# A fused attention and expert kernel: gate loads moved to ScalarE's queue, queries scaled ahead of the bonus sums, first keys decayed from PSUM, long idle products

## What is computed

```python
def _attn_ref(r, k, v, w, u):            # B, H, S, D = 4, 8, 768, 48
    state = zeros((B, H, D, D))
    for t in range(S):
        kt, vt, rt = k[:, :, t], v[:, :, t], r[:, :, t]
        cur = einsum('bhd,bhe->bhde', u[None] * kt, vt)
        y[:, :, t] = einsum('bhd,bhde->bhe', rt, state + cur)
        state = w[None, :, :, None] * state + einsum('bhd,bhe->bhde', kt, vt)

# x = y as 3072 tokens of 384. Expert layer: tokens with x @ w_skip > 0 go through
# the expert of their largest logit (x @ w_gate): x += gate * relu(x @ w1[e]) @ w2[e]
# Gated layer: out = ((x @ w1) * (x @ w2)) @ w3 @ w_out
```

## Time and profile before

| what | us |
|---|---|
| median of three runs | 617.81 |
| the profiled execution | 617.68 |
| its span, first to last instruction | 615.9 |
| TensorE busy (matmul rows) | 596.8 |
| VectorE, ScalarE, GpSimd busy | 292.5, 227.8, 144.7 |

### The profile page before, as it was taken

One profiled execution on the slowest core, in us unless ns is written; L12 is line 12 of the kernel. 1 busy time (PEld: TensorE's weight loads), 2 busy tenths in 40 slices (PEclk: granted clock), 3 DMA queues, 4 the chain that ended last, 5 costly groups with the idle time before them and its releaser, 6 DMA issues.

```text
span 615.9 us, 17326 instructions
## 1 busy us (share of the span) xinstructions
PE 596.8 (97%) x7377; PEld 532.8 (87%) x7377; DVE 292.5 (47%) x462; ACT 227.8 (37%) x409; POOL 144.7 (24%) x177
## 2 busy tenths in 40 slices
PE   6789999999999999999999999999999999999997
PEld 5689999766899999999688888888898888888886
DVE  5478889296577777774121231232232123223212
ACT  3156566434555555553231231232132122213212
POOL 7568877234144322221140000000000000000000
PEclk9799999999999999999999999999999999999999
DMA  7669997595567777640400030030011001001001
GB/s 134 127 138 186 185 184 188 212 308 189 168 267 268 282 273 254 212 159 20 160 15 0 1 103 0 1 103 1 1 44 60 0 1 52 0 1 51 1 0 52
DMA packets 103673, 67.77 MB, mean 110 GB/s; under 512 B 79124, under 2 KB 97688, under 8 KB 103632
## 3 DMA queue, kind: packets, MB, share of 16 engines
q1 hardware_dynamic: 76288, 57.89, 30.6%
q10 hardware_dynamic: 25552, 4.72, 4.1%
q0 software_dynamic: 1792, 4.58, 2.1%
HBM read 55.92 MB, written 12.19 MB: 111 GB/s over the span
## 4 chain that ended last, share of the span: by engine, by line
PE 50%; DVE 0%; ACT 0%; issue 0%
PE gl_pab L1511 32%; PE gl_po L1526 8%; PE p_pair L1526 8%; PE gl_pab L1499 1%; PE p_pair L93 0%; DVE gl_g_lo L1593 0%; DVE gl_g_sb L1591 0%; ACT gl_g_hi L1571 0%; ACT gl_a_sb L1568 0%; DVE gl_o_sb L1604 0%
## 5 line engine op out<-in xcount | busy, mean ns | idle before, releaser
L1591 DVE TENSOR_TENSOR gl_g_sb<-gl_a_sb,gl_pab 128x512 f32<-128x512 f32 x48 | 33.0, 688 | 186.3 <-ACT gl_a_sb L1568 186.3
L1511 PE MATMUL gl_pab<-gl_xT_hi,wm_lo 128*128 128x512 f32 x288 | 112.9, 392 | 0.0
L1511 PE MATMUL gl_pab<-gl_xT_lo,wm_hi 128*128 128x512 f32 x288 | 112.8, 392 | 0.0
L1511 PE MATMUL gl_pab<-gl_xT_hi,wm_hi 128*128 128x512 f32 x288 | 112.2, 389 | 0.0
L1568 ACT ACTIVATE gl_a_sb<-gl_pab 128x512 f32<-128x512 f32 x48 | 28.8, 599 | 183.9 <-PE gl_pab L1511 183.9
L1511 PEld LDWEIGHTS gl_pab<-gl_xT_hi,wm_lo 128*128 128x128 f32 x288 | 54.0, 188 | 11.4
L1511 PEld LDWEIGHTS gl_pab<-gl_xT_hi,wm_hi 128*128 128x128 f32 x288 | 54.1, 188 | 10.6 <-DVE gl_xT_lo L1598 0.3
L1511 PEld LDWEIGHTS gl_pab<-gl_xT_lo,wm_hi 128*128 128x128 f32 x288 | 54.0, 188 | 10.5
L1271 PE MATMUL ex_ph<-ex_xT_hi,ew_w_hi 128*128 128x224 f32 x192 | 52.9, 275 | 0.0
L1271 PE MATMUL ex_ph<-ex_xT_hi,ew_w_lo 128*128 128x224 f32 x192 | 52.7, 274 | 0.0
L1271 PE MATMUL ex_ph<-ex_xT_lo,ew_w_hi 128*128 128x224 f32 x192 | 52.7, 274 | 0.0
(11 more groups left out here) (204 smaller groups left out, 1220.7 us busy)
## 6 DMA issues: line engine op xcount, KB each, us to landing
w_in<-in_moe_w SPq DMA_DIRECT2D x8, 1536.0 KB, 8.2
ew_w_in<-in_moe_w SPq DMA_DIRECT2D x8, 1536.0 KB, 6.6
w_in<-in_moe_w SPq DMA_DIRECT2D x14, 512.0 KB, 7.4
k_in<-in_k SPq DMA_DIRECT2D x48, 96.0 KB, 3.1
v_in<-in_v ACTq DMA_DIRECT2D x48, 96.0 KB
r_in<-in_r SPq DMA_DIRECT2D x48, 96.0 KB, 3.1
w_in<-xbuf SPq DMA_DIRECT2D x12, 384.0 KB, 4.1
out<-gl_o_sb SPq DMA_DIRECT2D x12, 384.0 KB, 2.5
```

The lines of the kernel that those rows point to most:

```text
L1511: m = pe.matmul(p_ab[f % 2][w][:, :], a[:, w * KD + k, cols], b[t.slot][:, k, :], start=(k == 0 and n == 0), stop=(k == KD - 1 and n == 2))
L1591: dve.tensor_tensor(g_sb[f % 2][:, :], a_sb[f % 2][:, :], p_ab[f % 2][1][:, :], ALU.mult).then_inc(s_g, 1)
```

## The change

Five edits, all in the attention.

1. The two loads of `w_gates` go from SyncE's queue, behind tile 0's loads, to ScalarE's queue, directly behind its part of w.
2. TensorE's 24 transposes of `ident` become three f32 products of 512 columns into the same bank; `keep_warm` is gone.
3. `k_decay` of tile 0 multiplies by the powers in `p_Y` bank 0 itself (waiting for `s_kpT`). ScalarE copies bank 1 first, then waits until that decay is done (`s_kdec`) and copies bank 0; its load of the first values' second half now stands ahead of both copies. VectorE's wait at L552 is gone; it waits for both copies at tile 1.
4. In VectorE's list `rT_out` stands ahead of `bonuses`, in every step.
5. GpSimd waits for the bonus factors only behind its first product r * k.

```diff
@@ sync: load_rk
                 if at(t.c, t.j, 0):
-                    sp.dma_start(w_gates[:, :, 0:NL - 1], env["w_gate"].rearrange("(c p) e -> p c e", p=P)).then_inc(s_gates, 16)
-                    sp.dma_start(w_gates[:, :, NL - 1:NL], env["w_skip"].rearrange("(c p e) -> p c e", p=P, e=1),
-                                 allow_slow_non_contiguous=True).then_inc(s_gates, 16)
                     sp.dma_start(u_all[:, :, :].rearrange("p h d -> p (h d)"),
@@ tensor
             pe.wait_ge(env["s_iota"], 2)
-            keep_warm(pe, ident, p_K[:, 0, :], 24)
+            for _ in range(3):
+                pe.matmul(p_K[:, 0, :].rearrange("p (a b) -> p a b", b=P), ident[:, :], ident[:, :].unsqueeze(1).broadcast_to([P, 4, P]),
+                          start=True, stop=True, skip_group_check=True)
@@ scalar
             load_w(act, 1)
+            act.dma_start(w_gates[:, :, 0:NL - 1], env["w_gate"].rearrange("(c p) e -> p c e", p=P)).then_inc(s_gates, 16)
+            act.dma_start(w_gates[:, :, NL - 1:NL], env["w_skip"].rearrange("(c p e) -> p c e", p=P, e=1),
+                          allow_slow_non_contiguous=True).then_inc(s_gates, 16)
...
             def k_powers(a):
-                act.wait_ge(s_kpT, a + 1)
...
             zero(rT[1][:, :, :, :].rearrange("p j m c -> p (j m c)"))
+            issue_v(Tile(0, 0, 0), (1,))
+            act.wait_ge(s_kpT, 2)
+            k_powers(1)
+
+            act.wait_ge(s_kdec, BASE + 1)
             k_powers(0)
-            issue_v(Tile(0, 0, 0), (1,))
-            k_powers(1)
@@ vector
-            dve.wait_ge(s_kpow, 1)
...
-                if at(t.c, t.j, 2):
+                powers = k_pow[t.a][:, :, :]
+                if at(t.c, t.j, 0):
+                    dve.wait_ge(s_kpT, 1)
+                    powers = p_Y[:, 0, :].rearrange("p (h d) -> p h d", h=H)[:, :, 0:D]
+                if at(t.c, t.j, 1):
                     dve.wait_ge(s_kpow, 2)
-                dve.tensor_tensor(k_dec[:, t.slot, :, 0:D], k_in[t.slot][:, :, :], k_pow[t.a][:, :, :], ALU.mult).then_inc(s_kdec, 1)
+                dve.tensor_tensor(k_dec[:, t.slot, :, 0:D], k_in[t.slot][:, :, :], powers, ALU.mult).then_inc(s_kdec, 1)
...
-            schedule(dve, ((masks, 0), (states, -1), (bonuses, 1), (rT_out, 1), (x_out, -1), (k_decay, 2)), 2, 1, extra)
+            schedule(dve, ((masks, 0), (states, -1), (rT_out, 1), (bonuses, 1), (x_out, -1), (k_decay, 2)), 2, 1, extra)
@@ gpsimd
-            pool.wait_ge(s_u, 16)
...
                 wait(pool, s_rk, t.done())
+                if at(t.c, t.j, 0):
+                    pool.wait_ge(s_u, 16)
                 pool.tensor_tensor(ruk[t.pr][:, :, :], rk[t.pr][:, :, :], u_all[:, :, :], ALU.mult).then_inc(s_ruk, 1)
```

More of the change, by code:

```diff
@@ L24, in flat @@
     return x.rearrange("p a b -> p (a b)")
-def keep_warm(pe, ident, bank, n):
-    for _ in range(n):
-        pe.transpose(bank[:, 0:P], ident[:, :], ident[:, :])
 LINE = 1024
```

## The result

The changed kernel takes **618.28 us** (median of 20 runs, 617.11 to 620.64), the kernel before 617.14 on the same chip (20 runs). The ratio is 1.0017, with a 95% interval of 1.0009 to 1.0025: slower by 0.17%, 1.1 us, where I had forecast 0.3 us less. The forecast of 617.5 looks nearer than it is: it was worked out from a median of three runs, 617.81; from 617.14 it would have been 616.8. The profiled execution took 618.0 us, its span is 616.2.

What follows compares the result with a forecast made beforehand. TensorE, working almost without waits, was taken as the bound, its start held up by code fetches. From 617.68 us profiled, -0.3 from the borders and 0 elsewhere gave 617.4; the median, 0.13 above, made it 617.5, range 616.1 to 618.8.

Steps and rivals of the forecast that it cites:

- The holes are code, on a grid of some 250 rows, and move 36 rows with the products: TensorE before 35 us: "issue" holes of 1.24 to 2.44 us are waits for program code; borders fall 36 rows later.
- Rival D: TensorE's start: holes do not hang on code entry, the grid is chance; 617.4 or 617.1 us; chance 0.09.
- The products' own time, 0: TensorE's start: three long products take as long as the 24 transposes, 2.6 us at full clock; effect 0.
- The first block is released at 10.9 + 5.2 = 16.1: TensorE's start: first code block entered 0.34 us later, at 10.9, and released after an unchanged interval of 5.2 us.
- every later release moves with it: TensorE's start: later code releases also come 0.34 us later, with TensorE 36 rows further on, so that cancels.
- rival C: TensorE's start: loads fill the one quiet fetch interval, costing 1.3 us at most; 619.1 us; chance 0.17.
- my term of -0.3 us: Behind TensorE's first code hole: next border reached at 20.4 us instead of 20.7; bounds -0.7 and +0.5.
- A start that ends x us earlier ends the program x us earlier, and so far no queue stands between: From the start to the program's end: TensorE works almost without waits, so time won early carries through in full.
- Order of queries and sums 0: Attention start and loop: the 0.40 us hole before the first scores goes, but the code hole behind covers it; 0.
- gates 0: Start: gate loads leave SyncE's queue, later loads issued 1.1 to 1.2 us earlier; cost 0, bound +0.4.
- decay from PSUM 0: Tile 0's first key decay on VectorE: reading powers from PSUM costs as much as from SBUF, 0.55 us; effect 0.
- Rival B: Start: earlier loads leave DMA quieter during code fetches; 616.2 us with one shortened interval, 615.3 with two; chance 0.22.

Runs made afterwards that it cites:

- wide_loads: Kernel before, with key and retention-input loads of the first eight tiles in rows of 1,536 bytes instead of 192-byte pieces (other data): 615.72 us, ratio 0.9977.
- full_late_cheap: The change plus nine small products of 9 columns (36 rows) ahead of the first turn of a w3 piece: 617.19 us, ratio 0.9996.
- full_late_rows: The change plus 18 narrow transposes (36 rows) only at the first turn of a w3 piece: 617.73 us, ratio 1.0017.
- p_only: Kernel before with only the three long products in place of the 24 transposes: 617.52 us, ratio 1.0012.
- the best version: The change with the 24 transposes kept and four small products of 9 columns (16 rows) behind them: ratio 0.9969, on another chip 0.9968.
- full_third: The change once more, unaltered, on the chip of the kernels with late fillers: 617.92 us, ratio 1.0013.
- g_only: Kernel before with only the gate loads moved to ScalarE's queue: 616.43 us, ratio 1.0000.
- full_again: The change once more, unaltered, as a control against the kernel before: 618.01 us, ratio 1.0020.
- before_16_rows: Kernel before with four small products of 9 columns (16 rows) behind its 24 transposes and nothing else: 615.94 us, ratio 0.9973.
- borders_36_earlier: The change with the 24 transposes kept and 18 narrow transposes (36 rows) behind them: 615.79 us, ratio 0.9984.

## Why the prediction was wrong

Step by step, with the intervals between entry and release of a block, in us, from the traces of the kernels with one placing (`wide_loads`, which has other loads, and the single trace with borders 72 rows earlier are left out):

| borders | runs | first | last | mask 4 |
|---|---|---|---|---|
| old place | 7 | 4.59 to 5.15, mean 4.81 | 3.61 to 4.09, mean 3.91 | 37.7 to 41.0 |
| 36 later (the change) | 6 | 4.11 to 4.45, mean 4.26 | 4.13 to 4.62, mean 4.33 | 37.6 to 39.9 |
| 16 earlier | 3 | 3.81 to 4.03, mean 3.95 | 3.97 to 4.13, mean 4.03 | 36.7 to 37.4 |
| 36 earlier | 2 | 3.34, 3.68 | 4.13, 4.40 | 36.5, 37.8 |

- **The holes are code, on a grid of some 250 rows, and move 36 rows with the products: right.** In the twenty traces (those of both kernels and of all eighteen runs) the holes before 40 us that are marked "issue" and are over 0.5 us long end at the same counts of TensorE's rows, 423 to 427, 673 to 675, 923 to 925, 1171 to 1175 and 1421 to 1425, however many rows had been put in or taken away ahead of them. Rival D falls with them, and the 0.40 us before the scores was gone without a gain, as forecast.
- **The products' own time, 0: right.** They took 4.83 us against 4.50 and nobody waited; with the borders put back the change costs nothing (0.9997).
- **"The first block is released at 10.9 + 5.2 = 16.1" and "every later release moves with it": wrong, on both sides.** By the means of the table the first interval shrank by 0.55 us and the last grew by 0.42; the second, from 4.60 to 4.91, grew by 0.31. That the last grew is **rival C's mechanism**, which came true: the quiet stretch filled, DMA share 1.02 where one packet had been. Its size was a third of my 1.3 us. The third and the fourth interval shrank by 0.09 and 0.15, so the five together come out even. By the medians the start with the products and the new borders costs no more than before: `full_late_cheap` without its filler is 0.3 us under the kernel before, `full_late_rows` 0.5. That this is near my term of -0.3 us is luck: the term stood on a first release at 16.1 and on unchanged intervals, and both were wrong. The traces leave room for a small cost, since mask 4 comes at 39.1 us in the mean of the six and at 38.9 in that of the seven with the old place, each group spread over more than 2 us.
- **"A start that ends x us earlier ends the program x us earlier, and so far no queue stands between": the step that failed.** I had followed the borders only up to 35 us. Behind the attention they move too, and there a code fetch came to lie beside the store of the rows. All four runs with the late borders of the change have the wait for w3 (0.56, 0.22, 0.80 and 0.41 us in `p_only`) and a routing of 32.50 to 33.08 us, mean 32.78; 13 of the other 16 traces have 32.06 to 32.13 (before has 32.41, one of the best version 32.32, `wide_loads` 33.21). That is +0.7 us, and 1.0 us by the medians of `full_third` and `full_late_cheap`: most of the loss of 1.1. From the experts' first product to the end all twenty traces agree within 0.1 us, so nothing of the loss lies there. That the fetch slows SyncE's issue is inferred from their falling together in four traces of four, and from their going together in both runs whose late filler moved the fetch; no row names one as the other's releaser.
- **Order of queries and sums 0, gates 0, decay from PSUM 0: right.** 1.0002 and 1.0000 for the first two alone. For PSUM the row is 547 ns against 0.55 us; the larger fixed part that the Trainium skill gives for PSUM ("VectorE: DVE Perf Modes", the errata-adjusted cycle table) did not show here.
- **Rival B, loads out earlier and fetches quieter: no gain seen.** `g_only` is at 1.0000.
- **The clock had no step of its own in the prediction.** The change's trace has 13.6 us at 0.50 before 40 us, before has 6.8, and the five traces of kernels with borders 16 or 36 rows earlier have 3.4 in four, 10.2 in one. In the twenty traces each such stretch before 40 us begins inside a hole or up to 1.9 us behind one. Mask 4 goes with their sum: 36.5 to 37.8 us with 3.4 us at 0.50, 37.6 to 38.8 with 6.8, 37.3 to 39.7 with 10.2, 38.8 to 40.0 with 13.6, and 41.0 with 17.1. So the clock is likely part of the gain of those versions; no run separates it from the intervals. It doesn't carry the loss of the change: the mean granted clock over the runs was 0.9915 for `full_again` and 0.9920 for the kernel before beside it, and over all runs here 0.001 of clock goes with 0.1 us within one kernel (an estimate), against 1.0 us between the two.

The rule of the Trainium skill that crossing a block is mostly hidden ("Runtime: NRT & Kernel Launch", section "Instruction fetch mechanics") does not hold for this start, where borders leave holes of 0.3 to 2.9 us. The place of the holes matters as much as a hole does: by the place of the borders alone the same work takes 615.9 or 617.7 us (`before_16_rows` and the kernel before, on one chip). Why an interval is longer at one place than at another stays open.

## What to carry to other kernels

When an edit adds or takes away TensorE instructions ahead of a dense stretch of small products, it moves the borders of the program's blocks in everything behind: find the "issue" holes, count rows from one to the next, and follow the grid past the stretch that was edited, above all to places where a DMA issue is next on the path. Before such an edit is judged, run it with as many empty instructions as it took away; here that turned 1.0017 into 0.9997. And if TensorE waits for code at all, try two or three placings: four products of 9 columns ahead of the kernel before were worth 0.27%, where the five edits with the borders put back came out at 0.9997, and eighteen of them (with the other edits) cost 0.42%.

## What I had not expected of the hardware

- A code fetch far from the path still costs: beside it the issue of the store took 1.60 to 1.99 us in all four runs and 1.25 in the other traces. The load of w3 issued just ahead of it landed after 4.9 to 5.1 us in three of the four and after 4.1 in `full_third`, against 3.5 to 4.1 elsewhere.
- The time until the block's first packet after entry was 1.0 to 3.0 us in all traces, in the trace before 2.6 us at the first entry, with loads in flight, and 1.3 at the quiet last one; the wide loads changed it little (1.3 to 2.5).
- VectorE's q_pow product of 256 columns took 1.08 us at 8.60, where the earlier trace rows has no more than 0.55 for 384: GpSimd's first product now runs beside it (8.40 to 9.39). Before, it took 0.42 us. In eleven traces it started at 8.60 to 8.99, while that product ran, and in all eleven it ended 0.28 to 0.29 us after the product's end; in a twelfth (`borders_36_earlier`) it started at 9.31, 0.07 us before the product's end, and took its 0.42.
- Long products aren't denser than transposes in this start. Six rows took 4.83 us against 4.50 for 24, with each next weight load waiting 0.52 us for "issue". The rows stand 0.85 us apart, twice what late rows give (1.29 / 4 x 512 / 384 = 0.43), yet the trace shows a granted clock of 1.00 there, as the earlier trace rows does for the transposes. So the "lower clock" that the prediction read into the first of the 24 stands in their durations alone.
